# Rounding and splitting two sets of weights at other places of the steps, and half of their loads behind stores

## What is computed

```python
k_p, v_p = mean of k, v over groups of 8           # 8 x 8 heads, 576 -> 72 rows, 64 wide
x = softmax(q @ k_p.T / 8) @ v_p                   # gives x: 4608 x 512
def _moe_ref(x, w_in, w_out):                      # w_in 512 x 2048, w_out 2048 x 512
    h = x @ w_in
    g = h * (1.0 / (1.0 + np.exp(-h)))
    return (g @ w_out).astype(np.float32)
def _moe2_ref(x, w_in, w_out):
    h = x @ w_in
    relu6 = np.clip(h + 3.0, 0.0, 6.0)
    g = h * relu6 / 6.0
    return (g @ w_out).astype(np.float32)
```

## Time and profile before

| | us |
|---|---|
| time, median of 3 runs | 1703.68 (1703.26 to 1704.2) |
| the profiled execution's own time | 1705.6 |
| its span, first to last instruction | 1703.8 |
| PE busy | 1686.2 (99%) |
| DVE busy | 1040.7 (61%) |
| ACT busy | 726.5 (43%) |
| POOL busy | 351.9 (21%) |

### The profile page before, as it was taken

How to read it: one execution, slowest core, us unless ns; L and a number is a source line. 1 busy time by engine, 2 the same in 40 slices (tenths; PEclk the granted TensorE clock), 3 DMA queues, 4 the chain that set the end, 5 groups by cost and what they waited for, 6 DMA issues and landing times.

```text
span 1703.8 us, 27465 instructions
## 1 busy us (share of the span) xinstructions
PE 1686.2 (99%) x11096; PEld 1519.0 (89%) x11096; DVE 1040.7 (61%) x1568; ACT 726.5 (43%) x1183; POOL 351.9 (21%) x443
## 2 busy tenths in 40 slices
PE   8999999999999999999999999999999999999999
PEld 7888988998899999999999899999998899999998
DVE  7757656656656555555557655555557666666664
ACT  4655555555544533333334434343335433333332
POOL 6655534634206300000006200000006200000000
PEclk7899999999999999999999999999999999999999
DMA  8243333443212322222223211111112322222221
GB/s 211 77 119 102 109 97 106 113 120 101 76 47 99 124 75 75 75 75 75 77 79 130 91 53 54 53 53 54 44 61 88 117 77 79 77 78 78 78 79 49
DMA packets 129838, 145.83 MB, mean 86 GB/s; under 512 B 47536, under 2 KB 74416, under 8 KB 129712
## 3 DMA queue, kind: packets, MB, share of 16 engines
q1 hardware_dynamic: 79968, 127.95, 22.9%
q10 hardware_dynamic: 49744, 16.13, 3.8%
HBM read 96.86 MB, written 47.19 MB: 85 GB/s over the span
## 4 chain that ended last, share of the span: by engine, by line
PE 95%; DVE 3%; ACT 1%; issue 1%; DMA 0%; POOL 0%; ACTq 0%; DVEq 0%; POOLq 0%
PE zw L628 8%; PE zw L629 8%; PE zw L630 8%; PE xy L628 6%; PE xy L630 6%; PE xy L629 6%; PE acc L714 6%; PE acc L716 5%; PE acc L715 5%; PE acc L720 4%; PE acc L721 4%; PE acc L722 4%; PE att L720 4%; PE att L722 4%; PE att L721 4%; PE att L716 2%
## 5 line engine op out<-in xcount | busy, mean ns | idle before, releaser
L1217 DVE TENSOR_TENSOR g_lo<-g_raw,g_hi 128x1024 fp32r<-128x1024 f32 x144 | 194.8, 1355 | 9.4 <-ACT g_raw L920 9.4
L908 ACT COPY x_sum<-xy 128x256 f32<-128x256 f32 x144 | 52.4, 365 | 293.8 <-PE xy L630 293.5
L1182 DVE TENSOR_TENSOR x_sum<-xy,x_sum 128x256 f32<-128x256 f32 x144 | 60.5, 420 | 189.6 <-ACT x_sum L908 189.6
L628 PE MATMUL xy<-xr_hi,w1r_hi 128*128 128x256 f32 x576 | 166.0, 288 | 0.6 <-DVE x_sum L1182 0.6
L533 POOL TENSOR_TENSOR w_sum<-w_raw 128x256 f32<-128x256 f32 x16 | 16.6, 1036 | 715.9 <-DMA w_raw<-in_moe_w_in_dram 715.9
L630 PE MATMUL xy<-xr_hi,w1r_lo 128*128 128x256 f32 x576 | 163.4, 284 | 0.0
L629 PE MATMUL xy<-xr_lo,w1r_hi 128*128 128x256 f32 x576 | 163.3, 283 | 0.0
L714 PE MATMUL acc<-g_hi,w_hi 128*128 128x512 f32 x400 | 162.2, 405 | 0.0
L1206 DVE TENSOR_TENSOR g_raw<-zw,x_sum 128x512 f32<-128x512 f32 x144 | 99.0, 688 | 95.6 <-PE zw L630 95.6
L716 PE MATMUL acc<-g_hi,w_lo 128*128 128x512 f32 x400 | 156.4, 391 | 0.0
L715 PE MATMUL acc<-g_lo,w_hi 128*128 128x512 f32 x400 | 156.2, 390 | 0.0
(11 more groups left out here) (209 smaller groups left out, 4882.1 us busy)
## 6 DMA issues: line engine op xcount, KB each, us to landing
partial<-y_stage SPq DMA_DIRECT2D x72, 256.0 KB, 2.1
y_part<-partial SPq DMA_DIRECT2D x18, 1024.0 KB, 5.9
x_raw<-first_layer_t SPq DMA_DIRECT2D x18, 1024.0 KB, 7.8
x_raw<-attended_t SPq DMA_DIRECT2D x10, 1024.0 KB, 8.2
first_layer_t<-y_stage SPq DMA_DIRECT2D x36, 256.0 KB, 2.0
out_dram<-y_stage SPq DMA_DIRECT2D x36, 256.0 KB, 2.0
w_raw<-in_moe_w_in_dram SPq DMA_DIRECT2D x16, 512.0 KB, 4.2
kv_stage<-in_v_dram SPq DMA_DIRECT2D x56, 144.0 KB
```

Of the source, the lines that this page charges most:

```text
L628: nc.tensor.matmul(dst, s_hi[i], m_hi[i], start=first and i == 0, stop=False, skip_group_check=True)
L1217: nc.vector.tensor_tensor(g_lo[:, p], g_raw[:, p % 2], g_hi[:, p].bitcast(fp32), ALU.subtract)\
```

## The change

It alters where four things stand. `W1_ROUND_AT` goes from [4, 5, U+12, U+16] to [7, U, U+20, U+26], `W1_SPLIT_AT` from [U+18, U+21] to [U+22, U+29]. The second weights' rows are rounded at `W2_AT` instead of places 1 to 8. On SP's queue rows 0 to 3 are loaded two behind store 1 and two behind store 3, not all ahead of the stores, and rows 4 to 7 behind the loads of the partial sums and of x. In passes 2 and 3, at place 4, DVE does `chain_u(2)` before `split_g(0)` and `chain_c(2)` behind it. No instruction is added or removed.

```diff
--- before.py
+++ after.py
@@ -128,8 +128,10 @@
 
 
 
-W1_ROUND_AT = [4, 5, U + 12, U + 16]
-W1_SPLIT_AT = [U + 18, U + 21]
+W1_ROUND_AT = [7, U, U + 20, U + 26]
+W1_SPLIT_AT = [U + 22, U + 29]
+
+W2_AT = [1, 1, 7, U, U + 2, U + 4, U + 10, U + 14]
 
 
 def w1_splits(ps, p):
@@ -492,9 +494,6 @@
 
             for s in range(STEPS):
                 ps, blk = divmod(s, NB)
-                if ps and blk == 0:
-                    for f in range(4, NF):
-                        load_w2(ps, f)
                 if ps % 2:
                     load_part(s)
                 if s < FREE:
@@ -508,10 +507,14 @@
                 if blk == NB - 1 and ps + 1 < PASSES:
                     load_w1(ps + 1, 2)
                     load_w1(ps + 1, 3)
-                    for f in range(4):
-                        load_w2(ps + 1, f)
+                if ps and blk == 0:
+                    for f in range(4, NF):
+                        load_w2(ps, f)
                 for j in range(NK):
                     store_y(s, j)
+                    if blk == NB - 1 and ps + 1 < PASSES and j % 2:
+                        load_w2(ps + 1, j - 1)
+                        load_w2(ps + 1, j)
                 if blk == NB - 2 and ps + 1 < PASSES:
                     load_w1(ps + 1, 0)
                     load_w1(ps + 1, 1)
@@ -1161,8 +1164,9 @@
                         round_w1(0, 3)
                     if s == 0 and place in W2_FIRST_AT:
                         round_w2(0, W2_FIRST_AT.index(place))
-                    if ps and blk == 0 and 1 <= place <= NF:
-                        round_w2(ps, place - 1)
+                    for f in range(NF):
+                        if ps and blk == 0 and place == W2_AT[f]:
+                            round_w2(ps, f)
                     if blk == NB - 1 and ps + 1 < PASSES and place in W1_ROUND_AT:
                         round_w1(ps + 1, W1_ROUND_AT.index(place))
                     for j in range(NK):
@@ -1381,10 +1385,12 @@
                         if place in (2, 3, 6, 7):
                             swish_first(s, CHUNKS[place][1])
                             finish_h(s, CHUNKS[place][1])
+                        if place in (0, 1):
+                            chain(s, CHUNKS[place][1])
                         if place == 4:
+                            chain_u(s, 2)
                             split_g(s, 0)
-                        if place in (0, 1, 4):
-                            chain(s, CHUNKS[place][1])
+                            chain_c(s, 2)
                         if place == 5:
                             chain_u(s, 3)
                             split_g(s, 1)
```

## The result

The changed kernel takes 1721.18 us, median of 4 runs (1720.35 to 1721.23), against 1703.84 before: a ratio of 1.0099, 95% interval 1.0087 to 1.0112. It is slower, by 17.3 us; 1719.4 was forecast, in a range of 1703 to 1728. The steps of the changed kernel start at 516.77 (8), 558.71 (9), 606.05 (10), 899.63 (17), 941.57 (18), 990.47 (19), 1284.65 (26), 1326.83 (27) and 1379.72 (28) of its span of 1719.4 us. Its lines are 3 or 4 further on: L1186 is the old L1182 (`chain_u`), L1196 and L1198 are `chain_c`, L1221 `split_g`, L571 `split_w2`, L542 the last of `sums`.

What follows compares the result with a forecast made beforehand. PE, busy 99%, bounds the kernel. Steps 9, 18, 26 and 27 lose 5.9, 5.7, 0.4 and 11.4, together 23.4 against the old 7.7: +15.7 on 1703.7 gives 1719.4 us, range 1703 to 1728.

Steps and rivals of the forecast that it cites:

- What bounds it: PE is busy 99%; only its waits at three pass boundaries can change, at most 7.7 us to win.
- What goes: Old losses at the pass boundaries, 7.7 us, all vanish except some 0.4 in step 26.
- POOL's chain: Splits and sums of the first weights start 23.7 into steps 8 and 17, end at 44.7; in step 26 at 47.2.
- ACT's queue: Pair 3's rounding holds evacuations and next copy_p1; PE waits 3.2, 2.0 and 5.7 us in steps 9, 18 and 27.
- Second weights: PE waits in the units for late split rows: 0.5 us in step 9, 3.5 each in steps 18 and 27.
- Rows 6 and 7: Second weights' rows behind the x roundings: PE waits 1.3 and 0.7 us in step 18; just in time in step 9.
- Row 3: Second weights' row for unit 9, ready at 27.75 but wanted at 26.3 into step 18: costs 1.5 us.
- The clock: Long PE gaps bring the lower clock level: 2.0 us each in steps 9 and 27, nothing counted for step 18.
- The swap: chain_u(2) ahead of split_g(0) in 18 steps: chain_c ends at the same time, worth nothing in undisturbed steps.
- No change: Rival: POOL's first-weight work runs without meetings, ends at 38.5; only the second weights' 7.5 us remain: 1703.5 us; chance 0.1.
- Faster: Rival: second-weight splits fall between DVE's operations, x roundings aren't held, all 7.7 us go: 1696 to 1700; chance 0.1.
- More clock: Rival: three more falls to the low level (6.1 us) and first-weight sums 0.7 later in three steps: 1727.5; chance 0.1.

Runs made afterwards that it cites:

- the last version: Kernel before with SP's new order, W2_AT 1, 1, 6, 6, 7, 7, U, U, no swap, step 26's pairs 0 and 1 rounded inside place 6: 1697.3 us.
- the filled gaps: Changed kernel with 24, 15 and 43 spare matmuls, results unused, ahead of PE's wait in steps 9, 18 and 27: 1718.0 us.
- the second weights in the middle: Changed kernel with the second weights' rows rounded at places 1, 1, 6, 6, 7, 7, U, U: 1713.2 us.

## Why the prediction was right, point by point

**What bounds it.** Right: all of the difference lies in what PE waits for at the three pass boundaries, and in the 0.09 of each step below.

**What goes.** Right in size: step 26 lost 0.2 after the change. That nearly all of the 7.7 us can be had, by moving the same roundings, though to other places than the change did, is shown by the last version. The prediction's list of PE's waits left out a line, which is part of the 1.85 in steps 18 and 27 of the kernel before:

```profile
PE xy L628 <- DVE x_sum L1182: 0.6, 2, 0.3
```

**POOL's chain.** Begin at 23.7, forecast and measured; end at 44.9 and 47.4 where 44.7 and 47.2 were forecast. The step that carries the sum, DVE and POOL taking turns for all but 0.3 of each operation, was tested by making DVE's share small: the eight operations on x were to add 6.8 less 8 x 0.3 = 4.4, and without them the chain was 4.2 shorter. By the whole-instruction lock that the Trainium skill states (SBUF — State Buffer, "SBUF: two separate sides"), with X near 48 as the prediction worked out, step 9 would have waited some 6 us; it waited 2.95, so the trace doesn't bear out that form of the rule.

**ACT's queue.** The waits were 3.1, 2.1 and 5.4 (idle 2.95, 1.92, 5.26), forecast 3.2, 2.0 and 5.7. The path behind X, the end of POOL's sums, took 5.9 and not 6.2 (561.66 to 567.58); neighbours on ACT overlap by 0.1, which the sum left out. That it is the queue and not the data was shown by rounding later still and getting faster.

**Second weights.** 0.6 in step 9, forecast 0.5. In step 18 1.2, 1.3 and 0.7, together 3.2, against 1.5, 1.3 and 0.7; in step 27 also 3.2. Rows 6 and 7 are right. Row 3 is the only term that is off, since the low clock had made PE late already; with the old places of the first weights, where no fall comes before it, step 18 loses 3.5 at the units, as forecast.

**The clock.** Two falls of 2.0 each were counted, and step 18's left open. There were three, and they cost 1.3, 1.3 and 1.9, 4.6 in place of 4.0. The mechanism is shown by the filled gaps. The 2.05 was misread: it was all that step 26 lost beside the idle 1.83, but a wait costs more than its idle time, and the same step with the same gap at the full clock still loses 2.34. The low level cost 1.5 of the 3.88 there, not 2.05: matmuls come 0.22 apart in it and not 0.12, less than twice as long.

**The swap.** This step failed. "Ends `chain_c` at the same time; in undisturbed steps PE waits for neither" was taken from equal sums of durations. It ended 0.10 later, and the 0.17 between its end and PE's matmul was no slack but the handover: PE's step grew by nearly all of the 0.10. The term that the sums left out is the wait of `chain_c` for the split just ahead of it. It is 1.4 us in all.

**The total.** It is closer (2 us) than the terms are, and that is luck in part. The swap (1.4) and step 18's fall (1.3) were put at nothing; the falls of step 9 (2.0 for 1.3), the wait of step 27 (5.7 for 5.4), row 3 (1.5 for 1.2, twice) and step 26 (0.4 for 0.2) were put too high.

**Rivals.** "No change" asked for a chain without meetings of 14.8 us; with DVE's x operations nearly away it was still 17.0, of which 0.7 was a wait for a load and the rest of the difference is mostly DVE's two splits. "Faster" asked for row 3 split by 26.3, which the changed places don't give and place 6 does. "More clock" had five falls; there were three, since the gaps of 1.3 and less at the units brought none.

## What to carry to other kernels

To move a step later on an engine that takes its instructions in order, follow the slowest chain that it starts (here 21 us on POOL) to the instruction that waits for its end, and see what stands behind that one: it held three evacuations and the next step's first copy. Moves that look independent may need each other; each half of this one, taken without the new order of the loads, cost 24 to 26 us. And where PE is at 99%, its idle time at the few places where the pattern breaks is all that can be won; put work into the gaps in which the engine waits anyway, and compare step lengths, not totals.

## What the runs showed of the hardware that was not expected

- The same gap of PE may or may not be followed by the lower clock level. Behind the attention stage, gaps of 1.8 to 1.9 us were followed by it in step 26 of the kernel before, in step 18 of the changed one, in step 18 with the rounding of pair 3 behind the evacuations and in step 27 with DVE's short x operations, and weren't in step 26 with SP's new order alone, nor in step 18 with the second weights in the middle. Gaps of 1.7 and less never were, those of 2.9 and more each time.
- At the lower level PE's matmuls of 256 columns came 0.22 us apart (23 in 5.00 us, clock 0.50), against 0.12 at the full clock. A fall cost 1.3, 1.3 and 1.9 us in the changed kernel and 1.5 in the kernel before.
- A DVE operation that doesn't wait for the one ahead starts up to 0.09 us before its end. One that waits for the semaphore of the one just ahead starts 0.03 to 0.04 behind its end (`chain_c` behind `chain_u`, the first sums of x among themselves), and `chain_c` behind a split 0.13. An order of the same operations in which one such wait came to stand behind a split was 0.10 longer. Why the two waits differ isn't shown.
- A fall of the clock is partly paid back by the next wait: 82 spare matmuls kept the level up, which cost 4.6 us where it fell, and gained 3.2.
